# A fused attention and mixture-of-experts kernel: the gate logits move from VectorE and ScalarE to TensorE

## The reference

```python
logits = np.einsum('bsd,de->bse', x, w_gate)                 # 8 gates
local_gate = 1.0 / (1.0 + np.exp(-np.einsum('bsd,de->bse', x, w_local).squeeze(-1)))
for b in range(B):
    prev_e = -1
    for s in range(S):
        fresh_e = int(np.argmax(logits[b, s]))
        if s == 0 or local_gate[b, s] < 0.5: e = fresh_e
        else: e = prev_e if prev_e >= 0 else fresh_e
        prev_e = e
        ...                                                  # p = softmax of the logits
        out[b, s] = p[e] * (np.maximum(x[b, s] @ w1[e], 0.0) @ w2[e])
```

## Time and profile before

| what | us |
|---|---|
| median of 3 runs | 876.19 |
| lowest, highest | 875.71, 876.57 |
| the profiled execution | 876.57 |
| its span, first to last instruction | 874.5 |
| TensorE busy | 857.2 |
| VectorE busy | 406.8 |
| ScalarE busy | 342.2 |
| GpSimd busy | 154.7 |

### The profile page before, as it was taken

The page is one execution under the profiler, slowest core; times in us unless marked ns, Lnnn a source line. Parts: engine busy times, 40 slices in busy tenths (PEclk is TensorE's granted clock), DMA queues, the critical chain, the costliest instruction groups (busy, mean ns, idle before and its releaser), DMA issues.

```text
span 874.5 us, 19055 instructions
## 1 busy us (share of the span) xinstructions
PE 857.2 (98%) x6984; PEld 749.3 (86%) x6985; DVE 406.8 (47%) x732; ACT 342.2 (39%) x767; POOL 154.7 (18%) x158
## 2 busy tenths in 40 slices
PE   7999999999999999999999999989999999999996
PEld 6999999799899999789988889978778888888885
DVE  4667767421235425524545673672773342432221
ACT  4677667411126316413612531541332332432221
POOL 0311123485000000000000000039052121112111
PEclk9999999999999999999999999999999999999999
DMA  6654433126422101101201111422432341311111
GB/s 139 161 128 131 122 105 90 52 98 48 1 61 69 41 37 58 40 13 61 64 22 47 58 41 64 169 81 85 169 112 82 118 164 36 126 48 42 36 36 42
DMA packets 52469, 67.65 MB, mean 77 GB/s; under 512 B 29768, under 2 KB 29896, under 8 KB 52424
## 3 DMA queue, kind: packets, MB, share of 16 engines
q1 hardware_dynamic: 42552, 44.90, 19.0%
q10 hardware_dynamic: 6512, 11.64, 4.4%
q0 software_dynamic: 3360, 10.49, 3.7%
HBM read 57.58 MB, written 9.98 MB: 77 GB/s over the span
## 4 chain that ended last, share of the span: by engine, by line
PE 91%; DVE 5%; ACT 2%; issue 1%; another core or an unknown queue 1%; DMA 0%; POOLq 0%; SPq 0%; ACTq 0%; DVEq 0%
PE bank L1620 22%; PE bank L1622 22%; PE bank L1621 22%; PE bank L1534 7%; PE bank L1550 4%; PE bank L1507 4%; PE bank L1809 2%; DVE stage L1095 1%; PE bank L1495 1%; PE bank L1518 1%; PE bank L1672 1%; PE bank L1761 1%; ACT stage L917 1%; PE bank L1691 1%
## 5 line engine op out<-in xcount | busy, mean ns | idle before, releaser
L1064 DVE SCALAR_TENSOR_TENSOR hid_lo<-bank,hid_hi 128x384 fp32r<-128x384 f32 x96 | 53.5, 557 | 212.8 <-ACT hid_hi L893 212.8
L1620 PE MATMUL bank<-uT_hi,W 128*128 128x384 f32 x384 | 129.5, 337 | 0.3 <-DVE uT_lo L1083 0.3
L1622 PE MATMUL bank<-uT_hi,W 128*128 128x384 f32 x384 | 129.6, 338 | 0.0
L1621 PE MATMUL bank<-uT_lo,W 128*128 128x384 f32 x384 | 129.0, 336 | 0.0
L893 ACT ACTIVATE hid_hi<-bank 128x384 fp32r<-128x384 f32 x96 | 46.9, 488 | 186.0 <-PE bank L1622 178.1
L1620 PE MATMUL bank<-W,hid_hi 128*128 128x512 f32 x288 | 115.1, 400 | 3.5 <-DVE hid_lo L1064 3.3
L917 ACT ACTIVATE stage<-stage 128x512 f32<-128x512 f32 x135 | 84.6, 627 | 82.9 <-DVE stage L1095 76.4
L1622 PE MATMUL bank<-W,hid_lo 128*128 128x512 f32 x288 | 114.2, 397 | 0.0
L1621 PE MATMUL bank<-W,hid_hi 128*128 128x512 f32 x288 | 114.0, 396 | 0.0
L1095 DVE TENSOR_TENSOR stage<-rows,stage 128x512 f32<-128x512 f32 x135 | 93.4, 720 | 8.6 <-ACT stage L917 8.5
L1326 DVE TENSOR_TENSOR hT_lo<-bank,hT_hi 128x512 fp32r<-128x512 f32 x40 | 27.6, 691 | 105.4 <-ACT hT_hi L954 105.4
(11 more groups left out here) (274 smaller groups left out, 1410.9 us busy)
## 6 DMA issues: line engine op xcount, KB each, us to landing
rows<-in_moe_w SPq DMA_DIRECT2D x12, 1024.0 KB, 6.2
stage<-gate_rows ACTq DMA_DIRECT2D x38, 256.0 KB, 3.3
stage<-in_moe_w_ch SPq DMA_DIRECT2D x16, 512.0 KB, 3.9
qk_raw<-in_q SPq DMA_DIRECT2D x32, 144.0 KB, 3.0
vv<-in_v SPq DMA_DIRECT2D x32, 144.0 KB, 3.2
x_rows<-rows SPq DMA_DIRECT2D x6, 768.0 KB, 3.2
qk_raw<-in_k SPq DMA_DIRECT2D x30, 144.0 KB, 3.0
late_stage<-in_moe_w SPq DMA_DIRECT2D x4, 1024.0 KB, 6.3
```

Source lines behind the costliest of these rows:

```text
L1064: dve.scalar_tensor_tensor(out=hid_lo[:, n % 2], in0=bank[:, HB[n % 2], 0:TOK], scalar=0.0, in1=hid_hi[:, n % 2].bitcast(F32), op0=ALU.max ...
L1620: pe.matmul(dst, lhs_hi, rhs_hi, start=start, stop=False)
L1621: pe.matmul(dst, lhs_hi, rhs_lo, start=False, stop=False)
L1622: return pe.matmul(dst, lhs_lo, rhs_hi, start=False, stop=stop)
```

## The change

The gates of blocks 0 to 4 are no longer made by products and sums. They become six side jobs in the following block: four "x2T" jobs (three transposes each) at f = 2 to 5, "parts" at f = 6 and "logits" at f = 8. VectorE copies each of them out of its bank. The gate step, its buffers, its transfers and its semaphores go; those that waited for products or sums now wait for side jobs or for nothing. `x2T` uses `stage` up to column 1536, and `xg` lies behind it, so GpSimd fetches the first rows as soon as their ids are known. The rest of the diff joins two broken lines of `divide`.

```diff
         def side_jobs(b, f):
             jobs = []
+            if b >= 1 and 2 <= f < 2 + KC:
+                jobs.append(("x2T", b - 1, f - 2))
+            if b >= 1 and f == 2 + KC:
+                jobs.append(("parts", b - 1, 0))
...
+            if b >= 1 and f == 4 + KC:
+                jobs.append(("logits", b - 1, 0))
...
-        PICKED = LG * BLK * (NBLK // J)
+        PICKED = ("logits", NBLK // J - 1, 0)
...
-                    if gate_of(b, f) is not None:
-                        gate(gate_of(b, f))
...
@@ SP @@
-            sp.dma_start(gates_dram, w_gate.rearrange("d e -> e d"), allow_slow_non_contiguous=True)\
-              .then_inc(gates_turned, 16)
-            sp.wait_ge(gates_turned, 16)
-            sp.wait_ge(wst_split, W1P + W2P)
-
-            for k in range(2):
-                sp.dma_start(gate_row(k), gate_source(k)).then_inc(gate_loaded[k], 16)
...
-            sp.wait_ge(gate_product, LG * BLK * (NBLK - 2))
+            sp.wait_ge(side_out, jobs_before["x2T", NBLK - 2, KC - 1])
...
@@ GpSimd @@
-            pool.wait_ge(gate_product, PICKED)
+            pool.wait_ge(side_out, jobs_before[PICKED])
...
-            pre_split(0)
             pool.wait_ge(early_known, 1)
-            pool.wait_ge(gate_summed, LG * BLK * (NBLK - 1))
             fetch(early_id[:, 0:1], x2_dram[0:JT, :])
-            for n in range(1, 2 * EP):
+            for n in range(2 * EP):
                 pre_split(n)
...
@@ ScalarE @@
-            def gate(k):
-                b, g = k // LG, k % LG
-                for i in range(BLK):
-                    m = BLK * k + i
-                    act.wait_ge(gate_product, m + 1)
-                    act.activation(product(m), product(m), ACT.Copy, accum_out=logits[:, b * BLK + i, g:g + 1])\
-                       .then_inc(gate_summed, 1)
-                if k + 2 < LG * (NBLK - 1):
-                    act.dma_start(gate_row(k + 2), gate_source(k + 2)).then_inc(gate_loaded[k % 2], 16)
...
-                if n == 0:
-                    act.wait_ge(gate_product, LG * BLK * (NBLK - 1))
...
@@ VectorE @@
-            def gate(k):
-                b = k // LG
-                dve.wait_ge(gate_loaded[k % 2], 16 * (k // 2) + 16)
-                if k % LG == 0:
-                    dve.wait_ge(x2_ready, BLK * (b + 1))
-                for i in range(BLK):
-                    m = BLK * k + i
-                    if m >= 2:
-                        dve.wait_ge(gate_summed, m - 1)
-                    dve.tensor_tensor(product(m), rows[:, b * BLK + i, :], gate_row(k), ALU.mult)\
-                       .then_inc(gate_product, 1)
+                elif kind in ("x2T", "parts"):
+                    dve.tensor_copy(x2T[:, i], src[:, 0:TOK]).then_inc(side_out, 1)
+                else:
+                    dve.tensor_copy(logits[:, b * BLK:(b + 1) * BLK, :],
+                                    src[:, 0:BLK * LG].rearrange("p (t n) -> p t n", n=LG)).then_inc(side_out, 1)
...
-                    dve.wait_ge(gate_summed, PICKED)
+                    dve.wait_ge(side_out, jobs_before[PICKED])
...
-            dve.wait_ge(gate_summed, LG * BLK * (NBLK - 1))
...
@@ TensorE @@
-                else:
-                    pe.wait_ge(side_out, jobs_before["mix", b, BLK - 1])
+                elif kind in ("uT", "x2T"):
+                    if kind == "uT":
+                        pe.wait_ge(side_out, jobs_before["mix", b, BLK - 1])
+                    else:
+                        pe.wait_ge(x2_ready, BLK * (b + 1))
+                        if (b, i) == (0, 0):
+                            pe.wait_ge(wst_split, W1P + W2P)
                     for t in range(BLK):
                         mm = pe.transpose(dst[:, t * P:t * P + P], rows[:, b * BLK + t, i * P:i * P + P], ident[:, :])
+                elif kind == "parts":
+                    pe.wait_ge(side_out, jobs_before["x2T", b, KC - 1])
+                    if b == 0:
+                        pe.wait_ge(gates_set, 3 + KC)
+                    mm = gate_parts(dst)
+                else:
+                    pe.wait_ge(side_out, jobs_before["parts", b, 0])
+                    mm = add_up(dst)
                 mm.then_inc(side_done, 1)
...
-            pe.wait_ge(gates_set, 3 + KC)
```

More of the change, by code:

```diff
@@ L80, in moe_kernel @@
     x2_rows = x2_dram.rearrange("(j p t) d -> j p t d", p=P, t=T)
-    gates_dram = nc.dram_tensor("gate_rows", [E, DM], F32).ap()
     ctx = ExitStack()
@@ L328, in moe_kernel @@
         gates_loaded = sem("gates_loaded")
[L329 to L332, removed]
         gates_set = sem("gates_set")
@@ L484, in is_step, with ffn_order @@
             return isinstance(s, int) and s == n
[L486 to L499, removed]
+        def ffn_order(hidden, output, side, early=lambda stage: None, first_done=lambda: None):
             n = EARLY
@@ L910, in early @@
                     exp_shifted(0)
-            def gate(k):
-                b, g = k // LG, k % LG
-                for i in range(BLK):
-                    m = BLK * k + i
-                    act.wait_ge(gate_product, m + 1)
-                    act.activation(product(m), product(m), ACT.Copy, accum_out=logits[:, b * BLK + i, g:g + 1])\
-                       .then_inc(gate_summed, 1)
-                if k + 2 < LG * (NBLK - 1):
-                    act.dma_start(gate_row(k + 2), gate_source(k + 2)).then_inc(gate_loaded[k % 2], 16)
             attention_steps(act, step)
-            ffn_order(hidden, lambda b, f: None, side, early, gate=gate)
+            ffn_order(hidden, lambda b, f: None, side, early)
             def piece_hi(ord_, par, n):
@@ L1030, in divide @@
                         dve.wait_ge(n_done, OUTS * u + g + 1)
-                        dve.tensor_scalar(den[:, ts].unsqueeze(2), num_bank(g)[:, :, D:VW], EPS_DEN, None, ALU.add)\
-                           .then_inc(den_done, 1)
+                        dve.tensor_scalar(den[:, ts].unsqueeze(2), num_bank(g)[:, :, D:VW], EPS_DEN, None, ALU.add)                           .then_inc(den_done, 1)
                     dve.wait_ge(den_done, OUTS * u + OUTS)
@@ L1038, in divide @@
                         dve.tensor_tensor(rows[:, ds(T * j + ts.start, OT[g]), ds(D * h, D)], num_bank(g)[:, :, 0:D],
-                                          rden[:, ts].unsqueeze(2).to_broadcast([P, OT[g], D]), ALU.mult)\
-                           .then_inc(n_out, 1)
+                                          rden[:, ts].unsqueeze(2).to_broadcast([P, OT[g], D]), ALU.mult)                           .then_inc(n_out, 1)
                 if active(units, s, 3):
@@ L1080, in side @@
                     dve.tensor_tensor(col, src[:, 0:DM], col, ALU.add).then_inc(side_out, 1)
-                else:
+                elif kind == "uT":
                     dve.wait_ge(side_hi, hi_jobs[job])
@@ L1304, in _ @@
             steps(dve)
-            ffn_order(hidden, output, side, early, lambda: step(UNITS + 2, UNITS % 2, range(UNITS - 1, UNITS)), gate)
+            ffn_order(hidden, output, side, early, lambda: step(UNITS + 2, UNITS % 2, range(UNITS - 1, UNITS)))
             def piece_lo(ord_, par, n):
```

## The result

The kernel after takes 885.97 us (median of 4; 885.56 to 887.36) where the kernel before takes 876.06: a ratio of 1.0115, 95% interval 1.0098 to 1.0133. It is 9.9 us slower; 885.6 was forecast. The profiled execution took 884.51 us, with a span of 882.1.

The account below looks back on a forecast made before the run. TensorE's full instruction stream was taken to bound the kernel: 14.7 us of added jobs less 5.3 us of removed waits gave +9.4, so 885.6 us for the median. The forecast ran from 884.8 to 888.5, the range given from 884.0 to 888.9.

Parts of the forecast that it names:

- The bound: Feed-forward loop: TensorE's own stream, busy 98% of the span, sets the time; its waits on `hid_lo` total 3.3 us.
- The price of the jobs: Side jobs on TensorE: `x2T` 0.33 us each, `parts` 0.89, `logits` 0.73; 2.94 a block, 14.7 for five.
- The large stall: TensorE's wait at 574.73 to 578.21, from VectorE's product beside GpSimd's subtraction: 3.30 us plus 1.67 at lower clock, removed.
- The small wait: TensorE's matmul at 491.18, 0.36 us late from routing steps and gate products in one step; gone with the products.
- nothing hides this: The added jobs cost their full 14.7 us, as TensorE runs in order and the loop has no gap.
- The moves: Transfers, copies, expert loads and GpSimd's fetch shift at no cost; the first piece lands at 582, the fetch moves to 540.
- rival 1: Block 5: the port wait stays with `early_oh` as victim, margin 1.5 us; whole old stall back gives 890.9; chance 0.05.
- The sum: Whole kernel: +14.7 - 5.3 = +9.4 us, 886.0 for the profiled execution, 885.6 for the median.
- 2: The clock falls behind the added transposes in each block, 1.67 us times five, 8.4 us: 894; chance 0.03.
- 3: Products slow TensorE's pitch in 45 steps; over 0.21 us a step makes it faster; chance 0.02 faster, 0.01 no change.
- 4: Routing waits for logits until step 8 of block 3; a late logit would show before step 11; no price.
- The rule on transposes: Transposes don't count as work for the clock gate; taken at its word, the clock falls, though the trace showed none.

Follow-up runs that it names:

- e2: Kernel before, products and sums kept, plus TensorE's side work beside them without copies and with almost no waits; 888.81 us, ratio 1.0136.
- e1: Kernel before with GpSimd's first expert piece moved behind its fetch of the first rows; 876.25 us, ratio 1.0002.
- e3: Kernel before with the edits of e1 and e2 together, products and sums kept; 886.32 us, ratio 1.0117.
- b0: Kernel before, unchanged, a single execution for another look at the stall; 877.93 us.
- e0: Kernel after, unchanged, timed again beside the others on one chip; 885.68 us, ratio 1.0087.
- e4: Kernel after with `early_oh` at step 7 of block 5 instead of 6, where GpSimd subtracts; 885.42 us, ratio 1.0105.
- e5: Kernel before with GpSimd's pieces behind the fetch and the gate products one step earlier (steps 0 to 8); 872.19 us, ratio 0.9932.

## Why the prediction was right, point by point

- **The bound.** Right. TensorE's stream sets the time, and e2 shows that the price of the jobs is there without their copies and waits.
- **The price of the jobs.** 14.9 us against 14.7. `x2T` 0.33 as forecast: a group of three has no fixed part. `parts` 0.99 and not 0.89: the 0.1 ahead of the gate matmuls, which I had left to the upper bound, belongs to the group. `logits` 0.67 and not 0.73. The two errors nearly cancel.
- **The large stall.** Right in size: 4.97 forecast, 4.96 off block 5 (71.88 + 2.98 - 69.90). Right in cause: e1 ends it by moving GpSimd alone. The trace after could not have shown that, since there the products went and GpSimd moved at once.
- **The small wait.** The time was right in sign and too small, and the reason isn't the one that was needed. I put 0.36 us to the products' going. In e3 they stay and the wait goes all the same (what their going alone would do, no run shows); the jobs themselves fill it and other short waits of block 4, 0.9 us in all. The general statement "nothing hides this" failed by that much.
- **The moves.** Right: the first piece's cast at 582.14 (forecast 582), its subtraction at 584.13 (584), the fourth piece at 613.6 (614), the fetch at 539.4 (540). `early_oh` came 1.2 us earlier than worked out, at 579.8 (581.0), so the margin of rival 1 was 3.0 us and not 1.5.
- **The sum.** On the profiled executions it was +9.4 and is 884.51 - 876.57 = +7.9. The difference: +0.2 price and -0.54 block 4, which makes 9.0 for blocks 1 to 5, then -0.4 in block 0, -0.3 ahead of the loop and -0.7 behind it, and +0.35 outside the span. The -0.4 is not the change (b0 and e1 have the short block 0 too). Nor, it seems, is most of the -0.3 and -0.7: in e0's profile of the same kernel the loop starts at 179.66, 0.2 later than before and not 0.3 earlier, and the part of the span behind block 5 is 0.35 shorter and not 0.7. The median moved by 9.9, as the kernel after's timed executions are 1 to 3 us above its profiled one. So the 0.4 us by which 885.6 missed is luck in part; the sum itself was 1.5 us too high.
- **Rivals.** 1: did not happen, and e4 shows it harmless a step later. 2: 12 added transposes a block, and the clock granted stays at 1.00 through the loop; the time at stake did not appear. 3: 0.00 us a step, by e3. 4: TensorE waits for nothing in the loop but 0.3 us for `uT_lo`.
- **The rule on transposes.** The Trainium skill (TensorE: Matmul & The Clock Gate, Part 4: PE-mode transpose) says that they don't count as work for the clock gate in the way of other matmuls. In the loop and behind it, in groups of three to sixteen between large matmuls, no fall follows one. The falls of the first 50 us (b0 at 12.91, e5 at 15.01 and 42.31) lie in the attention stage, where short transposes, short matmuls and waits of up to 0.9 us take turns; e5's at 42.31 comes among transposes. Nothing here tells these causes apart, so the rule is neither refuted nor shown.

## What to carry to other kernels

When one engine is full, count what a change adds to its stream from start to start, second large instruction behind the group, and believe the idle time of the others only as far as it reaches that engine. Here 170 us of work were taken from two engines with room and gave back 5; those 5 were not load but one collision of GpSimd with a two-input VectorE instruction, which a reordering of a few lines removes without the 14.9 us (e5). When such a collision is moved, look at every two-input VectorE instruction in the new stretch, however small: what waits behind it sets the price.

## What the runs showed of the hardware

- A VectorE instruction with two SBUF inputs beside GpSimd's subtraction of 4.6 us waits for its end, whatever its own length: 0.69 became 5.1 us, 1.35 became 5.5, and 0.17 became 2.6 for nine elements. The last I had allowed 1.7 us at most; it cost 5.4, with the clock. A copy out of a bank is not held up (0.19 us at 608.47 in e1, beside the subtraction), nor is an instruction with one input in a bank and one in SBUF (`hid_lo`, 0.56 us beside subtractions).
- The cast, with one SBUF input, does the same: `early_oh`, begun in e2 while a cast ran until 582.93, took 2.17 us and not 1.35.
- It goes the other way round too: GpSimd's cast took 3.05 us and not 1.90 in e4 while `early_oh` held on, and its first subtraction took 5.60 (before) and 5.62 us (e2) and not 4.6, begun while `early_oh` ran.
- The Trainium skill (SBUF — State Buffer, SBUF: two separate sides) calls this an exclusive lock for the whole instruction. All these cases agree.
- A wait of TensorE of 2.4 us was followed by the lower clock for 6.8 us (e1), one of 3.1 us by 3.4 us of it, and the one of 1.6 us of e2 by 3.4 us. In e3 a wait of 1.6 us was followed by none. With the fall the stall of before cost 3.3 + 1.7 us, that of e1 5.4 us in all.
